# Values of the local windows: loads of 32 and 6 rows with all heads in one run, and GpSimd zeroing the half that a head does not own

## The reference, cut to what matters

```python
mask = np.abs(pos[:, None] - pos[None, :]) < factor        # factor = 4
scores = scale * np.matmul(q, k.transpose(0, 1, 3, 2))
scores = np.where(mask, scores, -1000000000.0)
...
out_local = np.matmul(attn, v)
return (out_up + out_local).astype(np.float32)
```

## Time and profile before

| | |
|---|---|
| median of three runs | 855.63 us |
| the profiled execution, its own time | 854.21 us |
| its span in the trace | 852.4 us |
| PE busy | 739.1 us (87%) |
| DVE busy | 437.0 us (51%) |
| ACT busy | 204.5 us (24%) |
| POOL busy | 61.2 us (7%) |
| DMA, mean over the span | 49.05 MB, 58 GB/s |
| V loads issued (line 349) | 80 |

### The profile page before, as it was taken

How to read it: one execution, slowest core, us unless ns; L and a number is a source line. 1 busy time by engine, 2 the same in 40 slices (tenths; PEclk the granted TensorE clock), 3 DMA queues, 4 the chain that set the end, 5 groups by cost and what they waited for, 6 DMA issues and landing times.

```text
span 852.4 us, 15400 instructions
## 1 busy us (share of the span) xinstructions
PE 739.1 (87%) x5956; PEld 547.4 (64%) x5956; DVE 437.0 (51%) x955; ACT 204.5 (24%) x409; POOL 61.2 (7%) x80
## 2 busy tenths in 40 slices
PE   1843554689989999899999999899999999999998
PEld 1721222457767677678767667677676777777776
DVE  7832466975445358464354477554263483112542
ACT  1211358512221111222221212122221122111101
POOL 2000021300011021000010020000110120000000
PEclk9999995589999999999999999999999999999999
DMA  9813323260130010441220001711300000000001
GB/s 289 242 47 92 90 71 126 56 152 16 40 83 4 1 57 29 142 77 32 49 49 2 29 29 47 180 26 31 82 13 1 1 28 29 1 2 1 1 12 45
DMA packets 58746, 49.05 MB, mean 58 GB/s; under 512 B 27504, under 2 KB 52208, under 8 KB 57584
## 3 DMA queue, kind: packets, MB, share of 16 engines
q1 hardware_dynamic: 50032, 31.59, 15.0%
q10 hardware_dynamic: 8640, 16.43, 5.6%
HBM read 43.29 MB, written 4.72 MB: 56 GB/s over the span
## 4 chain that ended last, share of the span: by engine, by line
PE 63%; SPq 15%; DVE 9%; issue 5%; DMA 5%; ACT 2%; POOL 1%; DVEq 0%; ACTq 0%; POOLq 0%
PE P L465 19%; PE Y L481 17%; SPq L349 10%; PE P L588 4%; PE Y L588 4%; PE Y L577 4%; PE A L490 3%; SPq L343 3%; DMA kl<-qk_win 2%; SPq L345 2%; PE A L436 2%; PE A L380 2%; PE A L538 1%; PE A L532 1%; DMA vl<-v_win 1%
## 5 line engine op out<-in xcount | busy, mean ns | idle before, releaser
L465 PE MATMUL P<-unT,w 128*128 128x288 f16 x1536 | 215.6, 292 | 8.1 <-issue 4.6
L481 PE MATMUL Y<-hT,w 128*128 128x288 f16 x1536 | 214.9, 286 | 1.5 <-DVE xT L1034 1.5
L1013 DVE SCALAR_TENSOR_TENSOR hT<-P,hT 128x288 f16<-128x288 f32 x128 | 58.4, 457 | 262.2 <-ACT hT L694 262.2
L465 PEld LDWEIGHTS P<-unT,w 128*128 128x128 f16 x1536 | 150.7, 100 | 54.9 <-issue 12.0
L481 PEld LDWEIGHTS Y<-hT,w 128*128 128x128 f16 x1536 | 144.9, 98 | 45.5 <-issue 7.0
L694 ACT ACTIVATE hT<-P 128x288 f16<-128x288 f32 x128 | 52.6, 411 | 198.4 <-PE P L465 198.4
L1049 DVE SCALAR_TENSOR_TENSOR gate<-xT,cw,gate 128x288 f32<-128x288 f32 x128 | 66.4, 519 | 4.5
L665 ACT ACTIVATE prob_or_un<-prob_or_un 73x288 f32<-73x288 f32 (+1 forms) x52 | 23.3, 448 | 171.8 <-DVE prob_or_un L884 171.8
L384 PE MATMUL Y<-mask_sb,idb_sb 128*128 128x304 bf16 x5 | 2.2, 431 | 35.4 <-DMA kl<-qk_win 35.4
L588 PE MATMUL P<-shared,wo 128*128 128x288 f32 x128 | 32.1, 409 | 0.7 <-DVE shared L1061 0.5
L588 PE MATMUL Y<-shared,wo 128*128 128x288 f32 x128 | 32.1, 409 | 0.5 <-DVE shared L1061 0.5
(11 more groups left out here) (141 smaller groups left out, 863.0 us busy)
## 6 DMA issues: line engine op xcount, KB each, us to landing
w<-w_ch ACTq DMA_DIRECT2D x8, 1024.0 KB, 8.7
vl<-v_win SPq DMA_DIRECT2D x80, 76.0 KB
kl<-qk_win SPq DMA_DIRECT2D x40, 140.0 KB, 3.7
ql<-qk_win SPq DMA_DIRECT2D x20, 256.0 KB, 5.1
pair_or_folded<-qk_pool SPq DMA_DIRECT2D x8, 580.0 KB, 5.0
pair_or_spectrum<-qk_pool SPq DMA_DIRECT2D x8, 580.0 KB, 5.5
out<-ot ACTq DMA_DIRECT2D x32, 144.0 KB, 1.8
x<-v_pool SPq DMA_DIRECT2D x4, 576.0 KB
```

The source lines that it names most:

```text
L465: last = mm(P[s % 2][:, 0:HN], w1s[:, k, f * 128:(f + 1) * 128, wt], unT[:, ut, k, ha * HN:(ha + 1) * HN], start=k == 0 and wt + ut == 0, ...
L481: last = mm(Y[d][:, 0:HN], w2s[:, f, d * 128:(d + 1) * 128, wt], hT[s % 3][:, ht, :], start=f == 0 and wt + ht == 0, stop=f == KF - 1 and ...
L1013: nc.vector.scalar_tensor_tensor(out=hT[s % 3][:, 1, :], in0=P[s % 2][:, 0:HN], scalar=0.0, in1=hT[s % 3][:, 0, :], op0=ALU.max, op1=ALU.s ...
```

## The change

Three things change. The V loads take all eight heads and the column of ones behind each head as one run: `vl` is laid out as rows x 2 offsets x 2 query halves x 8 heads x 65. The 38 rows of a half are fetched by two DMAs, one of 32 rows and one of 6, each for both offsets. Both heads' values now stand in both halves, so GpSimd multiplies, in place, the even heads' columns by a column that is 1 in the upper 38 rows and 0 in the lower, and the odd heads' by its opposite. PE waits for these products (`v_blocks`) and no longer for the load. The zeroing of `vl` goes; the small tiles are placed in one tile.

```diff
-        vl = [sb(f"vl{i}", [2 * LK, 4, 4, 2, D]) for i in range(2)]
+        vl = [sb(f"vl{i}", [2 * LK, 2, 2, H, D + 1]) for i in range(2)]
...
-                    sp.wait_ge(zeroed, 4)
+                    sp.wait_ge(zeroed, 2)
...
-                    for s in range(2):
-                        for j in range(2):
-                            sp.dma_start(vl[i][LK * j:LK * j + LK, 2 * s:2 * s + 2, :, j, :],
-                                         v_win[b, t, 32 * s:32 * s + LK, :, j:H:2, 0:D]).then_inc(ld_v[i], 16)
+                    for j in range(2):
+                        for lo, rows in ((LK - LQ, LQ), (0, LK - LQ)):
+                            src = v_win[b, t, lo:lo + 2 * LQ].rearrange("(s r) w h d -> r s (w h d)", s=2)
+                            sp.dma_start(vl[i][LK * j + lo:LK * j + lo + rows].rearrange("r s w h d -> r s (w h d)"),
+                                         src[0:rows]).then_inc(ld_v[i], 16)
...
-                    pe.wait_ge(ld_v[t % 2], 64 * (b * (3 - t % 2) + t // 2 + 1))
+                    pe.wait_ge(v_blocks, 2 * (NT * b + t + 1))
...
-                                      vl[t % 2][:, w // 2 + 2 * (w % 2), i, :, :], start=False, stop=True, skip_group_check=True)
+                                      vl[t % 2][:, w % 2, w // 2, 2 * i:2 * i + 2, 0:D], start=False, stop=True, skip_group_check=True)
...
+            def own_block(b, t):
+
+                v = vl[t % 2][:].rearrange("p s w (i j) d -> p j (s w) i d", j=2)[:, :, :, :, 0:D]
+                pool.wait_ge(ld_v[t % 2], 64 * (b * (3 - t % 2) + t // 2 + 1))
+                pool.sem_inc(passed, 1)
+                for j in range(2):
+                    nc.gpsimd.tensor_scalar(v[:, j], v[:, j], own_rows[:, j:j + 1], None, ALU.mult).then_inc(v_blocks, 1)
+
             def zero_rows(b, first):
 
+                for t in range(4):
+                    own_block(b, t)
                 for t in range(NT):
+                    if t == 3:
+                        pool.wait_ge(fold_a, 3 * b + 1)
+                        pool.sem_inc(passed, 1)
+                        own_block(b, 4)
                     if t == 2:
+                        pool.wait_ge(v_blocks, 2 * (NT * b + 4))
                         pool.wait_ge(x_sb, NT * b + 3)
...
-            for v in vl:
-                nc.gpsimd.memset(v[:], 0.0).then_inc(zeroed, 1)
+            nc.gpsimd.memset(own_rows[:, 0:1], 0.0)
+            nc.gpsimd.memset(own_rows[:, 1:2], 1.0).then_inc(rows_owned, 1)
+            pool.wait_ge(rows_owned, 1)
+            nc.gpsimd.memset(own_rows[0:LK, 0:1], 1.0)
+            nc.gpsimd.memset(own_rows[0:LK, 1:2], 0.0).then_inc(rows_owned, 1)
```

More of the change, by code:

```diff
@@ L73, in fused_kernel @@
         w1s, w2s = (w[:].bitcast(f16).rearrange("p k (f t) -> p k f t", t=2) for w in (w1, w2))
[L74 to L77, removed]
+        small = sb("small", [128, 2 * WCH + 4 + 2 + 1 + 2 + 2])
+        wmax = small[:, 0:2 * WCH].rearrange("p (i c) -> p i c", i=2)
+        wtop = small[:, 2 * WCH:2 * WCH + 4].rearrange("p (k i) -> p k i", k=2)
+        wscale, unscale = small[:, 2 * WCH + 4:2 * WCH + 6], small[:, 2 * WCH + 6:2 * WCH + 7]
+        mhalf, own_rows = small[:, 2 * WCH + 7:2 * WCH + 9], small[0:2 * LK, 2 * WCH + 9:2 * WCH + 11]
         wv = sb("wv", [128, KD, DM])
@@ L85, in fused_kernel @@
         fdft = sb("fdft", [128, 5, HE])
-        mhalf = sb("mhalf", [128, 2])
         pair_or_spectrum = sb("pair_or_spectrum", [128, 5 * HS])
@@ L174, in fused_kernel @@
         zeroed = sem("zeroed")
+        rows_owned = sem("rows_owned")
+        v_blocks = sem("v_blocks")
         normed = sem("normed")
@@ L1245, in _ @@
             pool.wait_ge(init, 2)
+            pool.wait_ge(rows_owned, 2)
             step(0, first=True)
```

## The result

The changed kernel takes 839.68 us (median of four runs, 838.18 to 842.80), the kernel before, measured beside it, 855.12. The ratio is 0.9828, 95% interval 0.9808 to 0.9848, a gain of 13 to 16 us. The forecast was 824.7, a gain of 31, with a range from 814 to 837. The direction was right; the gain was half of the forecast, and the time lies outside the range.

A forecast was written before the change was run, and what follows sets the result against it. The prediction took the first attention step to be bound by V's transfer and the loop by PE. Its sum was 854.2 - 26.3 (first step) - 5.9 (loop) + 1.3 (contention) = 823.3, with 1.4 to the median 824.7; range 814 to 837.

The forecast's parts named there:

- the product: GpSimd's multiplication of V by a 0/1 column, 76 x 1024: 1.5 us each, two make 3.0.
- V's data ahead of K in the cycle: First step: V's data takes 1.5 us at 410 GB/s, of which 0.1 falls ahead of K.
- V's landing in the last window: Window 4 of the first step: 1.6 us to issue V, about 3.6 to land behind weights and DFT tables.
- Mechanism: V's transfer at 36 GB/s bounds the first attention step; 32 rows spread over the engines as Q and K do.
- PE's 5.9 us of waits for K: In the loop, PE's six waits for K, issued behind V, vanish as V's issues fall from 7.27 to 1.6 us.
- GpSimd's late start: First arithmetic after GpSimd's reduction starts 6.85 us late; this moves to the first product, at 50.8, removing DVE's 6.13 us wait.
- the first V products: PE's start on V's products in the first step: 53.9 instead of 61.1, 7.2 us earlier.
- The cycle: First step, V of one window to V of the next: 12.3 us instead of 19.03; two cycles save 13.4.
- The last window: Window 4 to the stage's end: V lands about 85.5, products end near 88.7, DVE waits about 1.5 us in all.
- the last weight maximum: DVE's end of the first step's stage: 104.4 instead of 130.70, 26.3 us earlier (20.6 + 5.7).
- the 1.3 us allowed for contention: DVE slowed beside GpSimd's products at the stage's end and pooling at a turn's start: 1.3 us added, bounds 0 and 6.
- Rival 1: GpSimd (POOL) is the new gate, by 2.5 us products or late V for window 4: 832 to 836 us, chance 0.17.

The follow-up runs named there:

- e3: The changed kernel with V loaded as one DMA of 38 rows a half and offset, long runs and products kept: 922.83 us, ratio 1.0820.
- e9: The kernel before with only each V load split into 32 and 6 rows, 256 B pieces, no products: 831.93 us, ratio 0.9717.
- e1: The changed kernel with a host layout by head parity, each half loading only its own heads in 1 KB runs, no products: 822.77 us, ratio 0.9658.
- e4: The changed kernel with the last two loads of the second weight matrix issued three slots earlier: 835.21 us, ratio 0.9765.
- e2: The changed kernel, loads and all, without GpSimd's multiplication, so the halves are not zeroed: 834.05 us, ratio 0.9787.
- e5: The changed kernel with one product contiguous with a factor from memory, the other strided with a constant, halves not zeroed rightly: 841.40 us.
- e8: e2 with the lower half of the block fed from another window's rows, so V of the odd half is wrong: 832.43 us.
- e6: e1 with one small GpSimd multiplication right after its first reduction: 817.66 us, ratio 0.9563.
- e7: e6 with the earlier weight loads of e4: 818.77 us, ratio 0.9578.

## Why the prediction was off, point by point

Three terms of the sum were mis-sized: the product, V's data ahead of K in the cycle, and V's landing in the last window.

**Mechanism: right.** V's 38-row loads bound the first step, and the split into 32 and 6 lets them spread (e3, e9). PE's 5.9 us of waits for K in the loop went. GpSimd's late start moved to the first product (forecast 50.8, measured 51.83), and its fold no longer showed it.

**The product: mis-sized.** 1.5 us was taken, bound 2.5; it is 2.85, beyond the 2.5 that the prediction gave as a sign of being wrong. I argued from "one input" to the memset's rate; the two-input row, arithmetic on 512 elements, was the nearer one. That and the 1.0 of the start moved the first V products from 53.9 to 57.70: 3.8 us.

**The cycle: mis-sized.** 12.3 us was taken, 13.8 as the upper end; it is 14.7, together 4.8 us over two cycles. The step that failed is the price of V's data: 1.5 us at 410 GB/s, with 0.1 of it ahead of K. In window 2 of the changed kernel V's pieces run in the trace from 60.68 to 65.13 us, 4.45 us for 632 KB or 142 GB/s, and K lands 6.1 us after its issue, not 3.6; in e1, with half the bytes, it lands in 3.45. It is not only a queue behind V. The pieces of Q and K are themselves slow: the median is 53 ns for Q and 55 for K, against 27 and 29 in e1, and K's stay slow after V's last piece. I had priced the doubled data at the peak rate, and let nothing else slow by it.

**The last window: mis-sized.** From V's issue to the last weight maximum 23.9 us were forecast, 29.3 measured: 5.4 us. V landed 9.5 us after its issue, not 5.0, beside a megabyte of weights that the text named and did not price (e4). The products (6.1 us, not 3.0) follow, and one of GpSimd's folds stands behind them: DVE waited 6.83 us, not 1.2. The wait of 6.13 that the change removed was put back in another place. No run put that fold ahead of the products in GpSimd's program, though GpSimd stood idle for 4.65 us just before them; so how much of the wait is the order's and not the data's is open.

The three parts, 3.8, 4.8 and 5.4, are the whole difference between 104.4 and 118.47, 14.1 us with the roundings.

**The loop: 5.9 us forecast, about 4.4 found.** Turn by turn, from the scores of the first local window to those of the last, PE gains 2.5, 2.3 and 2.2 us, a little more than the 5.9. In the next slot it loses 0.9, 0.9 and 0.7: DVE, slowed by the products, is late with the residual. I had named this contention and put it at the stage's end and at the start of a turn, not here. e2, without products, keeps the whole gain. The loop and the 1.3 us allowed for contention thus differ by 0.2 us only.

**The execution itself.** The profiled run of the changed kernel lies 3.1 us above its median. At the start of its first and third turn PE ran longer at the lower of its two levels, 1.2 GHz; the granted clock is the last but two of the columns (changed kernel, then before, the third turn's first 26 us):

```profile
527.00:553.00 26.00, 24.24 (x174) 17.51 (x172) 13.65 (x25) 5.70 (x15) 7.26 (x3) 0.87 0.64 126
```
```profile
540.00:566.00 26.00, 25.41 (x198) 18.65 (x196) 15.20 (x29) 6.15 (x16) 0.00 (x0) 0.93 0.48 98
```

0.87 against 0.93 of full speed; PE lost 2.8 us there and 2.3 at the start of the first turn. The other turn does not show it, so I do not count it to the change, though no run settles that: other profiles have such a stretch too, with products (e5, 0.68 from 164 to 172 us) and without (e8, 0.62 from 159 to 167), where the kernel before has 0.79 at the same place. With these 5.1 us the parts add up: 12.2 in the first step and 4.4 in the loop, less 5.1, are 11.5, and the spans differ by 11.4.

**The range.** Rival 1 was what happened, all its parts at once: 3.8 us at the start where it had 2, cycles of 14.7 us where it had 13.8, and 5.4 us at the end, inside its 2 to 6. It had 0.17 and ended at 836; its cycle was worked out with the same too high data rate.

## What to carry to other kernels

Ask of every load how many rows its outermost dimension has: here 32 + 6 rows instead of 38 gained 24 us by themselves. Do not buy shorter issues with more bytes or with GpSimd arithmetic when a layout does the same: the host layout that keeps the halves apart (e1) gained 29 us, the change 15. When a transfer doubles, price it at the rate that a load of that shape shows with others around it; where no row has that shape, as here, widen the range. Then look at what is queued behind it, and at how fast that moves itself.

## What was not expected of the hardware

- GpSimd multiplies 1024 elements a partition in 2.8 us whether the run is contiguous or strided, the factor a constant or read from memory.
- The first arithmetic on GpSimd after its reduction starts 6.9 to 7.6 us late in most kernels, with the DMA engines all but idle (e6, 7.10) as with some 240 GB/s beside its first 4 us (the changed kernel, 7.60). It is 9.7 and 11.1 us with the early weights (e4, e7) and 14.4 us beside slow V loads (e3). That it waits for a transfer of its own would fit, but no run shows it.
- V's 4,160-byte pieces mostly take 161 ns up to the middle of a window in the changed kernel (window 2, to 61.7 us) and 250 to 700 ns after it, and Q's and K's small pieces behind them take twice their usual time. With 38 rows a load (e3) neither happens. Why is open.
